# A skipped turn in front of the PE loop, first loads one by one, and weights spread over the tiles

## The reference

```python
ret = scale * (q @ k.T) * Dmat          # Dmat: gamma[h] ** (i - j) for i >= j
x = (ret @ v)                           # to (4608, 512)
logits = x @ phi
d = exp(logits - max over tokens); d /= sum over tokens
slot_out[e] = relu((d.T @ x)[e] @ w1[e]) @ w2[e]
x = softmax(logits, over slots) @ slot_out
out = ((x @ fw1) * (x @ fw2)) @ w3 @ w_out
```

## Time and profile before

| what | us |
|---|---|
| median of 3 runs | 393.11 |
| lowest and highest | 389.04, 394.1 |
| the profiled execution | 394.4 |
| its span, first to last instruction | 392.6 |

### The profile page before, as it was taken

The page is one execution under the profiler, slowest core; times in us unless marked ns, Lnnn a source line. Parts: engine busy times, 40 slices in busy tenths (PEclk is TensorE's granted clock), DMA queues, the critical chain, the costliest instruction groups (busy, mean ns, idle before and its releaser), DMA issues. The chain is left out here.

```text
span 392.6 us, 16090 instructions
## 1 busy us (share of the span) xinstructions
PE 358.9 (91%) x7123; PEld 278.2 (71%) x7123; DVE 167.5 (43%) x329; ACT 125.2 (32%) x275; POOL 161.9 (41%) x155
## 2 busy tenths in 40 slices
PE   2683987898999999999999999899999999999996
PEld 1573876777878887774656555468878888888885
DVE  1321454556757765573013000699853323233320
ACT  1000121321433342222324220532734444434442
POOL 2521222322443542133546451298954554554530
PEclk9856799999999999999999999999999999999999
DMA  7898499897887886879999996057226655556222
GB/s 262 351 387 341 149 398 426 337 374 250 312 308 240 313 310 231 314 294 411 427 425 427 425 428 273 0 92 237 76 88 228 230 189 188 190 179 235 114 107 107
DMA packets 25914, 104.77 MB, mean 267 GB/s; under 512 B 2660, under 2 KB 5284, under 8 KB 16164
## 3 DMA queue, kind: packets, MB, share of 16 engines
q1 hardware_dynamic: 25892, 104.47, 71.1%
HBM read 94.14 MB, written 10.32 MB: 266 GB/s over the span
## 5 line engine op out<-in xcount | busy, mean ns | idle before, releaser
L561 POOL TENSOR_TENSOR pkg_sb<-pkg_sb,const_sb 128x512 f32<-128x512 f32 x36 | 37.5, 1042 | 106.4 <-DMA pkg_sb<-in_tiles 106.4
L623 POOL TENSOR_TENSOR feat<-c_sb 128x512 f32<-128x512 f32 x45 | 56.9, 1275 | 46.2 <-PE psum L991 44.3
L991 PE MATMUL psum<-m_hi,feat_hi 128*128 128x512 f32 x144 | 56.1, 390 | 0.3 <-DVE m_lo L1480 0.3
L991 PE MATMUL psum<-m_lo,feat_hi 128*128 128x512 f32 x144 | 56.0, 389 | 0.0
L991 PE MATMUL psum<-m_hi,feat_lo 128*128 128x512 f32 x144 | 56.0, 389 | 0.0
L428 DVE TENSOR_TENSOR feat_lo<-feat,feat_hi 128x512 fp32r<-128x512 f32 x34 | 27.2, 801 | 62.2 <-ACT feat_hi L1149 61.0
L1249 DVE TENSOR_TENSOR x_t<-psum,x_decay 128x512 f32<-128x512 f32 x36 | 24.9, 691 | 40.9 <-PE psum L693 40.9
L1007 ACT COPY x_nat<-psum 128x512 f32<-128x512 f32 x36 | 21.1, 586 | 65.8 <-PE psum L705 65.8
L648 PE MATMUL psum<-pkg_sb 64*64 64x64 f32 x1152 | 26.9, 234 | 16.2 <-POOL pkg_sb L561 7.3
L693 PE MATMUL psum<-weights_t,pkg_sb 64*64 64x64 f32 x1152 | 35.3, 238 | 5.7 <-issue 5.5
L1149 ACT CAST feat_hi<-feat 128x512 fp32r<-128x512 f32 x45 | 27.9, 623 | 39.0 <-POOL feat L623 39.0
(11 more groups left out here) (138 smaller groups left out, 569.0 us busy)
## 6 DMA issues: line engine op xcount, KB each, us to landing
pkg_sb<-in_tiles SPq DMA_DIRECT2D x34, 1024.0 KB, 4.9
unit_a<-in_units SPq DMA_DIRECT2D x16, 1024.0 KB, 13.8
c_sb<-c_rows SPq DMA_DIRECT2D x45, 256.0 KB
unit_x<-in_units SPq DMA_DIRECT2D x9, 1024.0 KB, 14.1
out<-out_sb SPq DMA_DIRECT2D x36, 256.0 KB, 2.0
fold_raw<-in_fold SPq DMA_DIRECT2D x6, 1024.0 KB, 9.3
unit_y<-in_units SPq DMA_DIRECT2D x5, 1024.0 KB, 12.3
unit_n<-in_units SPq DMA_DIRECT2D x4, 1024.0 KB, 12.2
```

Source lines behind the costliest of these rows:

```text
L561: nc.gpsimd.tensor_tensor(v_nat(n).rearrange("p (h d) -> p h d", h=HEADS), v_nat(n).rearrange("p (h d) -> p h d", h=HEADS), decay.unsqueez ...
L623: nc.gpsimd.tensor_tensor(feat[:, k, :], c_sb[:, s, x, :], c_sb[:, s, y, :], ALU.mult).then_inc(feat_ready, 1)
L991: last = mm(psum[:, OUT + b, :], x, y, start=(at == 0 and m == 0), stop=(at == 4 and m == 2))
```

## The change

PE's loop has ten turns instead of nine. Each of the four steps stands behind a branch `i > 0`, and turn 0 goes past all four to an else branch, in which tile 0's scores and update now stand, with the waits that were behind them. All tests of the turn's number are shifted by one.

SP issues the first halves with a wait between them: tile 1's first half when tile 0's first half is in, tile 1's second when tile 0's second is in, tile 2 when tile 1 is in, tile 3 when tile 0's scores are done. The expert units 0 and 1 come behind tile 3. The other eight weight loads come behind tiles 4, 7, 10, 13, 16, 19, 22 and 25: two fold loads, units 2 to 5, two fold loads. The fold loads of the first half of each matrix and of the second have a semaphore each.

```diff
-            for t in range(2):
-                load_first(t, 1)
-                load_first(t, 0)
+            load_first(0, 1)
+            load_first(0, 0)
+            sp.wait_ge(tile_loaded[0], 16)
+            load_first(1, 1)
+            sp.wait_ge(first_loaded[0], 16)
+            load_first(1, 0)
...
+            sp.wait_ge(first_loaded[1], 16)
             load_tile(2)
+            sp.wait_ge(scores_ready[0], 2)
             load_tile(3)
             load_first_unit(0)
+            load_first_unit(1)
+            weights = ([(load_fold, g, 0) for g in (0, 2)] + [(load_first_unit, u) for u in range(FIRST_WEIGHTS, 6)]
+                       + [(load_fold, g, 1) for g in (0, 2)])
             for n in range(SLOTS_IN, NTILES):
                 load_tile(n)
-                if n < SLOTS_IN + 2:
-                    load_first_unit(2 * n - 7)
-                    load_first_unit(2 * n - 6)
-                elif n == 8:
-                    load_first_unit(5)
-                elif n in FOLD_AT:
-                    at = FOLD_AT.index(n)
-                    load_fold(at // 2 * 2, at % 2)
+                if n % 3 == 1 and n // 3 <= len(weights):
+                    load, *which = weights[n // 3 - 1]
+                    load(*which)
...
-                    with pe.If(i < NTILES // SLOTS_IN - 1):
+                    with pe.If(i < NTILES // SLOTS_IN):
...
-                        with pe.If(i == dispatched_at(g) // SLOTS_IN):
+                        with pe.If(i == dispatched_at(g) // SLOTS_IN + 1):
...
-            with pe.Fori(0, NTILES // SLOTS_IN) as i:
+            def first_steps():
+
+                pe.wait_ge(first_loaded[0], 16)
+                pe.wait_ge(v_ready, 1)
+                scores(0)
+                update(0)
+                pe.wait_ge(first_loaded[1], 16)
+                pe.wait_ge(states_ready, 1)
+
+            with pe.Fori(0, NTILES // SLOTS_IN + 1) as i:
                 for r in range(SLOTS_IN):
-                    step(i, r)
+                    with pe.If(i > 0):
+                        step(i, r)
+                with pe.Else():
+                    first_steps()
...
-                if w == 0:
-                    act.wait_ge(fold_loaded, 16 * 4)
+                if w in (0, 4):
+                    act.wait_ge(fold_loaded[w // 4], 16 * 2)
```

More of the change, by code:

```diff
@@ L55 @@
 EARLY = 3
-FOLD_AT = (10, 11, 14, 15)
+FIRST_WEIGHTS = 2
 FOLD_HI_AT, FOLD_LO_AT = (18, 22, 26), (21, 23, 25, 27, 29, 31)
@@ L233, in build @@
         phi_loaded = sem("phi_loaded")
-        fold_loaded = sem("fold_loaded")
+        fold_loaded = [sem(f"fold_loaded{j}") for j in range(FT // 4)]
         fold_late_loaded = [sem(f"fold_late_loaded{j}") for j in range(FT // 4)]
@@ L449, in load_fold @@
                              fold_w[g, j].rearrange("p (j f) -> p j f", j=4)
-                             ).then_inc(fold_late_loaded[j] if g == 1 else fold_loaded, 16)
+                             ).then_inc(fold_late_loaded[j] if g == 1 else fold_loaded[j], 16)
             def load_first_unit(u):
@@ L755, in step @@
                 else:
-                    with pe.If(i > 0):
+                    with pe.If(i > 1):
                         logits(two_before)
```

## The result

The change is a little slower: 395.38 us against 392.49 (medians of 20 runs each), a ratio of 1.0081 with a 95% interval from 1.0053 to 1.011. The forecast was 385.4. The profiled execution after took 397.46 us with a span of 395.7, 3.1 more than the 392.6 of before. The ratio leaves out executions more than 1.5% above the fastest of their kernel, and the profiled one of the change lies just past that line, so its trace tells what costs what, and the medians tell how much.

The account below looks back on a forecast made before the run. PE, busy 91% of the span, was taken as bound by its slow first turn (code waits, low clock), then by loads. 9.7 + 0.7 - 2.7 = 7.7 us gain, 393.11 - 7.7 = 385.4 us; range 379.5 to 394.0.

Parts of the forecast that it names:

- The start: PE's first turn: tile 5's scores start at 32.4 us instead of 42.07, a gain of 9.7 us.
- F: Time of PE's first scores, 6.66 us before; taken as 15 us, with 10 and 28 kept as bounds.
- data bound early: Rival at the start: code is there when tile 1 is; 380.4 to 383.4 us, chance 0.15.
- The extra turn itself costs a few branches.: PE's loop: the added turn 0 was given no cost of its own in the sum.
- The weights: Loads inside the loop: eight weights and tile 4 cost about 10 us against 7.3 before, a loss of 2.7 us.
- the step behind it: PE's step after tile 5's scores: 3.42 us instead of 4.1, a gain of 0.7 us.
- The one with F = 20 and 2.7 us of gain: Rival at the start: all five code blocks come one after another; 390.4 us, chance 0.18.
- the slower one: Rival at the first real turn: blocks skipped in turn 0 are fetched again; 396.6 us, slower cases together chance 0.12.
- tile 3 hidden: First loads: tile 3 ready at 22 us, wanted at 25.6, so no wait, with 3.6 us to spare.
- the loop's end carried to the end: After the loop: an earlier loop end, 154 to 155 us instead of 162.4, moves the kernel's end with it.

Follow-up runs that it names:

- e13: The kernel before with only four weights in the loop, behind tiles 8, 12, 16 and 20, and six behind tile 35: 388.74 us, ratio 0.9887.
- e3: The change with the weights put back behind the tiles they stood behind before: ratio 1.0071 against the kernel before.
- e12: The change with its last three weights (unit 5 and two fold loads) moved behind tile 35: 391.19 us, ratio 0.9935 against the kernel before.
- e14: The change with only four weights in the loop, behind tiles 8, 12, 16 and 20, and six behind tile 35: 388.59 us, ratio 0.9872.
- e1: The kernel before with PE's loop of the change alone, all loads as before: 399.58 us, ratio 1.0154.
- e9: The change without the else branch, tile 0's scores made by the copy in step 3: ratio 0.9962 against the kernel before.
- e5: The change with one branch around all four steps instead of one around each: ratio 1.01 against the kernel before.
- e2: The kernel before with SP's load order of the change alone (first loads one by one, weights spread): ratio 1.0082.
- e4: The kernel before with only the spread of the weights, first loads at once: ratio 0.9991.

## Why the prediction was wrong

**The start, forecast 9.7 us, measured 3.8.** I took F = 15, in two or three rounds of blocks; it was 17.2. The "data bound early" rival was out, and the blocks nearly came in a row. Two smaller terms were missing beside it. Between first and second scores I had 2.0 us; it was 4.3, since PE also goes back through the loop's end and waits 2.3 us there. And tiles 4 and 5 were late by 1.57 and 1.40, where I had 1 to 2 in all. Against that the clock was up sooner: without these two waits the four steps took 13.9 us (16.85 - 2.97) where I had 15.4. 2.2 + 2.3 + 3.0 - 1.5 make, but for rounding, the 5.9 by which 38.3 misses 32.4. It is the largest of the misses: five blocks' arrival, the loop's own way back, and the tiles behind them were each taken too short. The mechanism (code ahead of the work, the clock at its higher level from the first turn's second step on) was right, only its size was off.

**"The extra turn itself costs a few branches."** This step failed. I costed the added branches once, for the added turn, but the branch with its else stands in every turn. 0.37 us in each of the seven heads behind tile 5 is 2.6 us. A sum over every turn of what the edit puts at the turn's end would have asked the question, although no row of before had the answer.

**The weights, forecast 2.7 us lost.** The sum was about right (forecast about 10 us; 10.4 from tile 5 on). But I compared it with 7.3 before as if both were for the same number of loads: before, only the last five of the ten weights stand among the tiles of those waits. The other five lay under the first turn, where no tile was waited for. They were cheap there, not free: with none of them there, e13 has code waits of 2.72, 1.43, 1.26 and 2.55 us in its first turn, 8.0 us against 11.2. The change takes those waits away and has to pay for three of these weights in front of tiles 4 and 5 and for more of them later; e3 shows that putting them back behind the tiles of before doesn't avoid it. Behind tile 6 the waits grew by 1.7 us (9.0, without the head of tile 33, against 7.3), and in the profile 2.6 us came on top by the clock, which fell for one step behind each of the two longest stops. I had no term for that.

Behind tile 6's scores: 2.6 of heads, 1.7 of waits, 2.6 of clock, together 6.9 of the 8.0 us by which the stretch to tile 35 is longer (120.65 against 112.68); the rest has no one place. With the 3.8 us gained by tile 5, 0.85 in the step behind it (4.14 to 3.29, forecast 0.7) and 0.2 at the end, the 8.0 make the 3.1 us of the two spans.

**The rivals.** The one with F = 20 and 2.7 us of gain was nearest at the start, and the slower one named the wrong place: the skipped blocks were there. That its 396.6 us is close to the 395.38 measured is luck. None said that PE's own turn grows, or that the cover of the early weights goes. What is late next when a stall goes I asked only of tiles 3 and 4.

**What held.** No code wait over 0.3 us inside turn 1, the clock up before 25.25 us, tile 3 hidden, seven of the nine late waits from tile 5 on behind a weight (the 0.47 us ahead of tile 28 and the head of tile 33 are not), and the loop's end carried to the end within 0.2 us.

## What to carry to other kernels

A stall at the start of a kernel may be the cover under which transfers cost little. Before it is taken away, list what runs beneath it, and find those transfers another place: here the next part of the kernel took three weight loads for nothing (e12), which was worth 1.5% on top of the change, and six of them for 2 us (e13, e14), while the skipped turn itself paid only in one of four places of the weights. And count what an edit of a loop adds to every turn, not only what it adds once.

## What the runs showed of the hardware

- TensorE's code came in packets of 16 KB, and how fast depended on the data queue: with the first loads one by one the first scores came at 17.2 us (e3), with four tiles in the queue at once at 21.4 (e1, the same loop and weights). Fewer jumps brought the first scores forward (10.69 us in e9, 7.07 in e5), and the code waits behind them took most of it back in e9 and more than all in e5: tile 5's scores came at 37.70 and 43.08 us against 38.30.
- Code that was loaded stayed: the later turns of a loop over at least five blocks waited 0.2 us for it in all. A jump past all four steps left blocks out, and PE waited for them in turn 1 (e5: waits of up to 2.9 us there, 16 packets in place of 14).
- An else branch with 32 matmuls' code in it cost 0.4 us at each turn of the loop that jumped over it (3.96 to 4.00 us over a turn's head instead of 3.59), and about half of that went with it (3.82 in e9). Branches that lead to the next instruction cost nothing that shows (3.59 with and without). The Trainium skill (Advanced Engine Details and Errata, "Control Flow Timing") gives about 51 ns for a branch and 108 ns for a compare and branch, far below that.
- After stops of 1.86 and 2.08 us in the change the granted clock was at its lower level for part of the next step (0.64 and 0.69 in the mean), and so it was after 1.58 us in e2 (0.63) and after 1.74, 1.88 and 1.84 us in e4 (0.66, 0.63, 0.63). After 1.57, 1.49 and 1.40 us in the change it stayed at 1.00, and so it did after 2.00 us in e14, 2.04 in e2, 2.08 in e5 and 2.11 in e12. The length of the stop alone does not decide it.
